# A band-and-pooled attention ahead of two MLPs on one core: where the later units' pooled scores stand, and their place in two orders of work

## The reference

```python
def _attn_ref(q, k, v):                      # (4, 8, 576, 64) each
    factor, scale = 4, 1.0 / np.sqrt(D)
    q_d, k_d, v_d = means over groups of 4 positions      # 144 positions
    out_up = np.repeat(softmax(scale * q_d @ k_d.T) @ v_d, factor, axis=2)
    mask = np.abs(pos[:, None] - pos[None, :]) < factor   # a band of 7 keys
    out_local = softmax(where(mask, scale * q @ k.T, -1e9)) @ v
    return out_up + out_local

x = attention as (2304, 512)
h = relu(x @ w_in); x = (s * h * h + b) @ w_out           # 512 -> 2048 -> 512
out = ((x @ w_a) * (x @ w_b)) @ w_out2                    # 512 -> 1536 -> 512
```

## Time and profile before

| | |
|---|---|
| median of 3 runs | 976.09 us (976.05 to 976.31) |
| profiled execution, device time | 976.43 us |
| its span, first to last instruction | 974.6 us |
| boot stage | up to about 40 us |
| first MLP with units 4 to 31 | about 40 to 553 us |
| second MLP | from 553 us |
| PE busy | 952.4 us, 98% |
| DVE busy | 614.2 us, 63% |
| ACT busy | 471.3 us, 48% |
| POOL busy | 203.1 us, 21% |
| chain that ended last | PE 91%, DVE 5%, ACT 2%, issue 1%, DMA 1% |

### The profile page before, as it was taken

One profiled execution on the slowest core, in us unless ns is written; L12 is line 12 of the kernel. 1 busy time (PEld: TensorE's weight loads), 2 busy tenths in 40 slices (PEclk: granted clock), 3 DMA queues, 4 the chain that ended last, 5 costly groups with the idle time before them and its releaser, 6 DMA issues.

```text
span 974.6 us, 18320 instructions
## 1 busy us (share of the span) xinstructions
PE 952.4 (98%) x6902; PEld 900.3 (92%) x6902; DVE 614.2 (63%) x1087; ACT 471.3 (48%) x1112; POOL 203.1 (21%) x216
## 2 busy tenths in 40 slices
PE   6799999999999999999999999999999999999997
PEld 5699999999999999999999999999999999999996
DVE  5788665656565656555646656666866667766642
ACT  4667554545454545454534544444634345644432
POOL 2200211001210011200021033333333333333310
PEclk9599999999999999999999999999999999999999
DMA  8345211111301122101041142222442222422201
GB/s 199 100 138 159 75 51 26 41 48 38 98 15 26 39 74 63 46 18 48 11 154 34 46 141 66 66 66 66 130 141 77 75 66 65 130 66 65 74 24 66
DMA packets 129352, 71.41 MB, mean 73 GB/s; under 512 B 63248, under 2 KB 120304, under 8 KB 129264
## 3 DMA queue, kind: packets, MB, share of 16 engines
q1 hardware_dynamic: 128224, 69.94, 25.1%
q10 hardware_dynamic: 1040, 0.29, 0.1%
HBM read 60.76 MB, written 9.44 MB: 72 GB/s over the span
## 4 chain that ended last, share of the span: by engine, by line
PE 91%; DVE 5%; ACT 2%; issue 1%; DMA 1%; SPq 0%; ACTq 0%; DVEq 0%
PE bank L712 27%; PE bank L662 20%; PE bank L648 20%; PE bank L728 15%; PE bank L616 2%; PE bank L561 1%; PE bank L599 1%; PE bank L609 1%; PE bank L567 1%; DVE wx L1048 1%; PE bank L528 1%; PE bank L541 1%; PE bank L585 1%; ACT sml L771 1%; DVE stat L984 1%
## 5 line engine op out<-in xcount | busy, mean ns | idle before, releaser
L712 PE MATMUL bank<-wx 128*128 128x384 f32 x1512 | 287.5, 336 | 0.6 <-ACT u L950 0.6
L712 PEld LDWEIGHTS bank<-wx 128*128 128x128 f32 x1512 | 267.1, 188 | 14.7 <-ACT u L950 0.9
L662 PE MATMUL bank<-g_hi,wx 128*128 128x288 f32 x1024 | 231.8, 302 | 0.0
L648 PE MATMUL bank<-wx 128*128 128x288 f32 x1536 | 228.8, 298 | 1.5 <-ACT relu L862 1.5
L648 PEld LDWEIGHTS bank<-wx 128*128 128x128 f32 x1536 | 210.2, 188 | 5.0 <-ACT relu L862 1.7
L1199 POOL TENSOR_TENSOR raw<-raw 128x256 f32<-128x256 f32 x144 | 143.1, 1013 | 303.4 <-DVE wx L1119 263.4
L662 PEld LDWEIGHTS bank<-g_hi,wx 128*128 128x128 f32 x1024 | 171.4, 188 | 3.5 <-issue 0.3
L728 PE MATMUL bank<-wx 128*128 128x512 f32 x648 | 173.3, 394 | 0.8 <-DVE wx L1119 0.8
L662 PE MATMUL bank<-g_lo,wx 128*128 128x288 f32 x512 | 151.5, 296 | 0.0
L728 PEld LDWEIGHTS bank<-wx 128*128 128x128 f32 x648 | 119.3, 188 | 17.1 <-DVE wx L1119 1.3
L862 ACT ACTIVATE relu<-bank 128x288 f32<-128x288 f32 x128 | 52.4, 409 | 149.6 <-PE bank L648 149.4
(11 more groups left out here) (70 smaller groups left out, 890.7 us busy)
## 6 DMA issues: line engine op xcount, KB each, us to landing
raw<-in_moe_w_b SPq DMA_DIRECT2D x72, 128.0 KB, 2.3
raw<-in_moe_w_a SPq DMA_DIRECT2D x72, 128.0 KB, 2.3
raw<-in_moe_w_out SPq DMA_DIRECT2D x36, 256.0 KB, 2.8
vnat<-in_v SPq DMA_DIRECT2D x32, 144.0 KB
o_transposed<-o_sb SPq DMA_DIRECT2D x8, 576.0 KB, 3.2
o_raw<-o_transposed SPq DMA_DIRECT2D x6, 768.0 KB, 6.1
out<-y SPq DMA_DIRECT2D x18, 256.0 KB, 2.3
natq<-in_q SPq DMA_DIRECT2D x63, 72.0 KB, 2.1
```

The lines of the kernel that those rows point to most:

```text
L648: mm = nc.tensor.matmul(HB[:, 0:HALF], wi(w, kd, f), xs(x, c % 2)[:, kd], start=(kd == 0 and j == 0), stop=(kd == KD - 1 and j == 2))
L662: mm = nc.tensor.matmul(ACC[o][:, 0:HALF], wo(w, f, o), g[:, slot % GB, :], start=(f == 0 and j == 0), stop=(f == F1 - 1 and j == 2))
L712: mm = nc.tensor.matmul(dst, left(w, n, a, kd), right(x, i)[:, kd * HC:(kd + 1) * HC], start=(opens and kd == 0 and m == 0), stop=(kd == K ...
```

## The change

It concerns units 4 to 31.

- The pooled scores of head `e` go to columns 320 to 463 of bank `e`, behind the local scores, instead of bank 2 (`sp_place`). On PE all six local products come first, heads in the order 0, 1, and the two pooled products last, without the wait between them.
- `scores(u)` no longer waits for `o_taken`; `turn_pooled(u)`, the next to write bank 2, does.
- `turn_k(u)` and `turn_q(u)` of a following unit wait for `ep_ready` (the pooled exponentials have been read out of banks 0 and 1) where they waited for `masked` (the local scores have been read). A leading unit's `turn_q` keeps its wait for `k_taken`. The last unit's `turn_local` gets a wait for `ep_ready`.
- `minima` waits for `sp_ready` instead of `sl_ready`, and takes the pooled minima and their shift ahead of the local minima.
- On ACT `exp_pooled` stands at tick 2, ahead of `exp_local`, instead of tick 3.

```diff
+        def sp_place(u, e):
+            at = bank[0:GH, c_bank(u), e * G:(e + 1) * G] if alone(u) else bank[0:GH, e, SP_AT:SP_AT + G]
+            return at
...
@@ turn_k and turn_q
-                    pe.wait_ge(masked, u)
+                    pe.wait_ge(ep_ready, u)
...
@@ scores
                     pe.wait_ge(ptl_taken, u)
-                    if u > PAIRS:
-                        pe.wait_ge(o_taken, u)
...
+                else:
+
+                    for w in range(GW):
+                        for e in (0, 1):
+                            mm = local_scores(e, w)
+                    mm.then_inc(sl_ready, 1)
+                    for e in (0, 1):
+                        mm = pooled_scores(e)
+                    mm.then_inc(sp_ready, 1)
...
@@ turn_pooled
                 pe.wait_ge(pp_ready, u + 1)
+                if u > PAIRS:
+
+                    pe.wait_ge(o_taken, u)
...
@@ turn_local
                 elif u + 1 < NU:
                     pe.wait_ge(q_taken, u + 2)
+                else:
+                    pe.wait_ge(ep_ready, u + 1)
...
@@ ACT, attention
                 for u in at_tick(g, 6, 2):
+                    if not alone(u):
+                        exp_pooled(u)
                     exp_local(u)
...
                 for u in at_tick(g, 6, 3):
-                    exp_pooled(u)
+                    if alone(u):
+                        exp_pooled(u)
...
@@ DVE, minima
-                dve.wait_ge(sl_ready, u + 1)
+                dve.wait_ge(sl_ready if alone(u) else sp_ready, u + 1)
...
+                if not alone(u):
+                    local_minima()
```

More of the change, by code:

```diff
@@ L38 @@
 WARM = 6
+SP_AT = 320
 GB = 3
@@ L555, in scores @@
                     pe.wait_ge(ptl_taken, u)
-                    if u > PAIRS:
-                        pe.wait_ge(o_taken, u)
                 def pooled_scores(e):
                     rows = slice(e * D, (e + 1) * D)
-                    return nc.tensor.matmul(bank[0:GH, c_bank(u), e * G:(e + 1) * G], kits[kit(u)]["pooledq"][rows, :],
+                    return nc.tensor.matmul(sp_place(u, e), kits[kit(u)]["pooledq"][rows, :],
                                             pooledk[rows, p, :], start=True, stop=True)
@@ L569, in local_scores @@
                                             kT[rows, key:key + WK], start=True, stop=True)
[L572 to L578, removed]
+                if alone(u):
+                    pooled_scores(0).then_inc(sp_half, 1)
+                    for w in range(GW):
+                        for e in (1, 0):
+                            mm = local_scores(e, w)
+                    mm.then_inc(sl_ready, 1)
+                    pe.wait_ge(sp_half, u + 1)
+                    pooled_scores(1).then_inc(sp_ready, 1)
+                else:
+                    for w in range(GW):
+                        for e in (0, 1):
+                            mm = local_scores(e, w)
+                    mm.then_inc(sl_ready, 1)
+                    for e in (0, 1):
+                        mm = pooled_scores(e)
+                    mm.then_inc(sp_ready, 1)
             def turn_pooled(u):
                 pe.wait_ge(pp_ready, u + 1)
+                if u > PAIRS:
+                    pe.wait_ge(o_taken, u)
                 for e in range(2):
@@ L982, in minima, with local_minima @@
                 nc.vector.tensor_tensor(x, src, rows, ALU.subtract).then_inc(masked, 1)
[L983 to L986, removed]
+                def local_minima():
+                    dve.wait_ge(masked, u + 1)
+                    nc.vector.tensor_reduce(mnl(u), kits[kit(u)]["sml"][:, :, 0:WK], X, ALU.min).then_inc(mnl_ready, 1)
+                if alone(u):
+                    local_minima()
+                    dve.wait_ge(sp_ready, u + 1)
+                if alone(u):
+                    src = bank[0:GH, c_bank(u), 0:2 * G].rearrange("p (e c) -> p e c", e=2)
+                else:
+                    src = bank[0:GH, 0:2, SP_AT:SP_AT + G]
                 nc.vector.tensor_reduce(mnp(u), src, X, ALU.min).then_inc(mnp_ready, 1)
```

6 lines of the change are left out of this document (4 added, 2 removed).

## The result

The changed kernel takes **981.88 us** (median of 5 runs, 981.56 to 982.49) against 976.09 us before (975.66 to 976.62): a ratio of 1.0059 (95% interval 1.0048 to 1.0069), slower by 5.8 us. 985.1 us was forecast, 9.0 us more than before, in a range from 979.5 to 989.5. The direction and the places were right; the rise was forecast half too large (9.0 for 5.8).

A forecast was written before the change was run, and what follows sets the result against it. The prediction took PE's own gap-free list to bound the first stage; its terms, 5.6 + 1.9 + 0.4 + 1.7 - 0.7 = 8.9, say 9.0 us, gave 985.1 us, range 979.5 to 989.5.

The forecast's parts named there:

- PE as the bound, each wait lost in full: First stage: PE's own list bounds it, so any new wait on PE is lost in full, with no later wait returning it.
- term 3: Units 4 to 6, with the weight splits: 0.7 us lost in unit 4, 0.5 us each in 5 and 6; 1.7 us.
- What ACT does after the change: ACT's list: pooled exponentials first push local exponentials, g_hi and key copy back by 0.82 us; the next relu keeps its time.
- Term 1: Query turn waits for the key copy in the 12 units whose follower leads: 12 x 0.47 = 5.6 us.
- the prediction's own sign: Key copy on ACT: the first term is wrong unless it starts 2.9 us behind the first exponential (2.05 before).
- Term 2: Pooled transposes wait for POOL's product in 12 units whose follower doesn't lead: 12 x 0.16 = 1.9 us; last unit 0.4.
- Term 4: Unit 8's scores no longer wait 0.68 us for o_taken; the moved wait delays nothing on PE: -0.7 us.
- Term 5: The block of scores on PE keeps its 0.95 us despite the new order of passes: 0 us.
- Only one of terms 1 and 2: Rival: only one of the two waits, at query turn or pooled transposes, is real: +2.5 to +4 us; chance 0.08.
- The delay spreads: Rival: late g_lo or relu reaches PE too, half a microsecond in all 28 units: 990 us and more; chance 0.07.
- no change: Rival: the turns on PE have slack that start times hide, a queue of work ahead: 976 us; chance 0.05.
- faster: Rival: fewer waits at the scores' head close the "issue" gaps: -5.5 us, 970.6 us; chance 0.04.

The follow-up runs named there:

- Run 8: Kernel before with its banks, scores and waits; pooled minima ahead of local ones, pooled exponentials at tick 1, ahead of relu: 976.76 us, ratio 1.0002.
- runs 3 and 5: Changed kernel, pooled reciprocal ahead of the local sum on DVE: throughout, 982.79 us; only in units from 9 whose follower doesn't lead, and the last, 981.12 us.
- run 1: Kernel before with only the change's DVE and ACT orders; its banks, score order and waits stay: 983.33 us, ratio 1.0068.
- run 9: Changed kernel, pooled exponentials at tick 1, ahead of relu, from unit 5 on; unit 4 keeps local minima and exponentials first: 975.69 us, ratio 0.9986.
- run 7: Changed kernel with the pooled exponentials one tick earlier on ACT (tick 1), ahead of relu: 976.44 us, ratio 1.0.
- run 2: Changed kernel with a leading unit's key copy directly behind the local exponentials on ACT, ahead of g_hi: 979.15 us, ratio 1.0025.
- run 6: Changed kernel, pooled reciprocal ahead of the local sum on DVE, POOL's v sums held back until the local product is done: 981.53 us, ratio 1.0052.

## Why the prediction was right, and where its sizes were off

- **PE as the bound, each wait lost in full**: right from unit 8 on. Run 8 shows it from the other side: with no producer late there, units 8 to 30 take as long as before. In unit 4 it was wrong (term 3).
- **What ACT does after the change** is the step that was mis-sized: 0.82 us, from the first start to the end of the last accumulator read. The next activation doesn't wait for that read, and the push is 0.71 us. In the earlier trace rows relu starts at 144.95, just behind the read, which looked like a queue in which the read counts; but the 12 matmuls that relu needs end then too (started 143.08, 1.83 us long, so 144.91). Unit 5 of the kernel before, where relu wasn't waiting for PE, shows the overlap (timeline, ACT):

```profile
61.43 0.19 ACT L762 ACTIVATION_READ_ACCUMULATOR smp<-bank,stat 72x1 f32 x1
61.52 0.39 ACT L862 ACTIVATE relu<-bank 128x288 f32<-128x288 f32 x1
```

- **Term 1**, 12 x 0.47 = 5.6 us: measured 12 x 0.37 = 4.4. The push is 0.11 us shorter, and the load follows the copy after 0.12 us instead of 0.14; 0.03 us is lost behind the turn, which I had not counted. By the prediction's own sign (2.9 us behind the first exponential; measured 2.76) this term was off in its size. The place, the count and "nearer the matmul than the load" held. That the key turn isn't late held too (143.08, 0.14 behind the pooled exponentials).
- **Term 2**, 12 x 0.16 = 1.9 us: measured 12 x 0.06 = 0.7. A small difference of larger numbers: with 0.71 for 0.82 it is 0.05. For the last unit 0.4 was forecast, 0.34 measured. The list of waits was to name it some 14 times. It names it in units 4 and 31 only: the waits of 0.05 us don't show in it, so the distances are the proof, and runs 3 and 5, which remove them.
- **Term 3**, 1.7 us: measured 1.0. In unit 4 the pooled transposes do come 0.71 us later behind the local ones, but these come 0.26 us earlier (8.59 us behind the scores' first matmul for 8.85), and 0.2 us comes back behind the pooled ones. The prediction had no later or earlier wait there that could give anything back; PE's wait for relu, which the earlier trace rows leaves out, stands ahead of the local transposes and ends that much earlier. Units 5 and 6 lose 0.39 and 0.34, not 0.5 each.
- **Term 4**, -0.7 us: measured -0.75, and run 1, where the wait stays, loses it again.
- **Term 5**, 0: right, 0.95 us before and after, the 23 gaps "issue" as they were (3.8 us). The Trainium skill, "TensorE: Matmul & The Clock Gate", Part 3 (Packing small matmuls), says that matmuls start and end strictly in program order. The starts in the earlier trace rows contradict it, and the 2 us that the prediction worked out from it for pairing the pooled passes didn't come.
- **The sum**, 9.0: measured 5.8. Nearly all of the 3.2 us is in terms 1, 2 and 3, too large by 1.2, 1.2 and 0.7; for the first two it is the one mis-sized step, 0.11 us in each of 24 units. No error in it made up for another.
- **The rivals.** "Only one of terms 1 and 2" came nearest by its size (+4), but both are there; and the measured rise is 5.8. "The delay spreads" is refuted by units 11 to 30, which lose nothing elsewhere; "no change" by the distances; "faster" by the gaps that stayed. The sentence that a faster kernel needs the pooled exponentials in ACT's idle time ahead of relu is what run 9 shows.

What stays open: why the clock fell in run 7. PE's idling in unit 4 isn't enough. The profiles of the changed kernel and of runs 1, 2 and 8 have PE busy for 2.76 or 2.77 us from 48 to 52 us too, and the clock stays at 1.00 in all of them. Nor is the long low clock in boot enough: run 2 has it at 0.50 from 15 to 40 us, like run 7, and the idling as well. The second group of run 7 has the lower mean clock in all five runs, but a fall of 3.4 us accounts for only 0.002 of the difference of 0.01 or more, the rest lies elsewhere (in boot, in the one of them that has a profile), so the mean doesn't show that the fall was in all five. That it was is argued from the times. Nor is the split peculiar to run 7: three of run 8's 11 runs (978.23 to 978.72 us, mean clock 0.982 to 0.984, the others 0.987 to 1.000) and one run of the kernel before in each of the three sets of measurements (2.2 to 3.1 us above its median, at 0.982 or 0.983, which others of its runs have too) stand apart. So run 9 shows 1.1 us gained and no second group in 11 runs, not that its edit keeps the clock up. In its trace the gain needs no clock: 0.76 us is unit 7's, and 0.27 comes from units 4 to 6.

## What to carry to other kernels

Where one engine is the bound and gap-free, a reorder on another engine is priced by the slack of each thing queued behind it: list what the moved piece is put ahead of, take for each the time from its end to the first instruction that wants it (loads too), and compare with the push from start to start, not from start to end. Look for idle time before the place first; one tick earlier the same reorder cost nothing from unit 8 on. And an edit that brings GpSimd forward has to be checked for the VectorE work that it then lies beside.

## What the runs showed of the hardware beyond that

- **An accumulator read lies beside the next activation.** The read of 0.20 us at 142.74 ends 0.11 us after the next activation has started. Two exponentials of 72x144 with their reads delay what follows by 0.71 us, not 0.82.
- **VectorE and GpSimd side by side.** The product of two tensors in SBUF, 96x612 fp32, takes 0.79 us alone and 1.69 to 1.70 beside GpSimd's sums; the square 128x288 0.51 and 0.98. GpSimd's first sum took 1.28 to 1.29 us there, 1.44 in run 6 and 1.53 in the changed kernel, so over the product it was VectorE that paid; its second took 1.16 to 1.17 us there, 0.83 in run 6 and 1.60 in the changed kernel, beside VectorE's split of weights. The Trainium skill, "GPSIMD Engine Reference", Specifications, has the SBUF interfaces of GpSimd shared with VectorE, with contention where an instruction of VectorE has two SBUF inputs. The product has them, and the trace agrees; the page gives no size.
- **Matmuls on different halves of the partitions start out of the program's order**: a local pass of head 1 starts at 136.80 us, and head 0's second pooled pass, which precedes it in the program, at 136.97. Neither order of the passes within the scores is worth anything: 0.95 us both ways.
- **The granted clock fell to 0.57 over 4 us** in run 7, after 4 us at 1.00 in which PE was busy 2.77 us. In the changed kernel, with 2.76 us, and in before, with 3.41, it stayed at 1.00. So nearly the same idling went with a fall and with none.
